# Smaller attention state, later weight loads, and the last stage's convolution split around the gate products

## What is computed

```python
# attention, b, h, block by block
out = (q @ k.T * Dmask) @ v + (q * lam_pow) @ kv_state
kv_state = lam ** block * kv_state + (k * rev_pow).T @ v
# experts: x is the attention output, e the token's expert
out[b, s] = p[e] * (np.maximum(x[b, s] @ w1[e], 0) @ w2[e])
# last layer
gate_pre = sum(conv_w[k] * xp[:, k:k + S, :] for k in range(5))
y = (sigmoid(gate_pre) * (x @ w_val)) @ w_out
```

## Time and profile before

| | |
|---|---|
| Time, median of 3 runs | 379.99 us (378.61 to 380.9) |
| The profiled execution | 382.69 us, span 380.9 us |
| PE busy | 358.0 us, 94% of the span |
| DVE, ACT, POOL busy | 236.8, 176.3, 70.7 us |
| Mean granted PE clock | 0.969 of full speed |

### The profile page before, as it was taken

How to read it: one execution, slowest core, us unless ns; L and a number is a source line. 1 busy time by engine, 2 the same in 40 slices (tenths; PEclk the granted TensorE clock), 3 DMA queues, 4 the chain that set the end, 5 groups by cost and what they waited for, 6 DMA issues and landing times.

```text
span 380.9 us, 6692 instructions
## 1 busy us (share of the span) xinstructions
PE 358.0 (94%) x2512; PEld 327.7 (86%) x2512; DVE 236.8 (62%) x511; ACT 176.3 (46%) x297; POOL 70.7 (19%) x66
## 2 busy tenths in 40 slices
PE   6997999979999999999999999999996993999997
PEld 5896999868998989899898998989995892998986
DVE  6776689986572672837647285571801889989420
ACT  1336256411263554636456274462620982955422
POOL 4426699872000000000000000000006600000000
PEclk9999699988999999999999999999999898799999
DMA  7999999336209476494755937464014600010113
GB/s 231 420 409 403 401 312 331 103 134 210 96 5 354 142 275 218 156 353 130 262 201 200 341 120 284 157 238 148 2 57 118 195 22 0 28 57 35 51 54 110
DMA packets 30761, 70.10 MB, mean 184 GB/s; under 512 B 2320, under 2 KB 2832, under 8 KB 30224
## 3 DMA queue, kind: packets, MB, share of 16 engines
q1 hardware_dynamic: 26192, 59.25, 43.9%
q0 software_dynamic: 1920, 6.29, 5.0%
q10 hardware_dynamic: 2624, 4.22, 3.0%
HBM read 55.08 MB, written 14.68 MB: 183 GB/s over the span
## 4 chain that ended last, share of the span: by engine, by line
PE 81%; DMA 8%; DVE 5%; ACT 3%; issue 2%; POOL 0%; SPq 0%; DVEq 0%; POOLq 0%
PE bank L1115 76%; DMA w_raw<-w 5%; DVE gate L1058 2%; PE bank L1268 2%; PE bank L1343 1%; PE bank L1168 1%; DMA y_slots<-y_out 1%; DMA x_all<-y_slots,gather_u 1%; DMA lam_all<-lam 1%; DVE decay L795 1%; PE bank L1185 1%; ACT gate L690 0%; ACT w_sp L676 0%; ACT w_raw L692 0%; ACT state_dec L565 0%
## 5 line engine op out<-in xcount | busy, mean ns | idle before, releaser
L1115 PE MATMUL bank<-w_sp,h_sp 128*128 128x512 f32 (+1 forms) x480 | 106.7, 380 | 0.0
L1115 PEld LDWEIGHTS bank<-w_sp,h_sp 128*128 128x128 f32 x480 | 86.3, 188 | 16.4
L1115 PEld LDWEIGHTS bank<-x_sp,w_sp 128*128 128x128 f32 x768 | 93.2, 192 | 0.9 <-issue 0.3
L1115 PE MATMUL bank<-x_sp,w_sp 128*128 128x256 f32 x768 | 93.8, 283 | 0.1
L898 DVE TENSOR_TENSOR w_sp<-w_raw,w_sp 128x1024 fp32r<-128x1024 f32 x60 | 70.8, 1222 | 12.3 <-ACT w_sp L556 12.1
L556 ACT ACTIVATE w_sp<-w_raw 128x1024 fp32r<-128x1024 f32 x68 | 68.6, 1057 | 16.8 <-PE bank L1115 13.6
L975 DVE SCALAR_TENSOR_TENSOR h_sp<-bank,h_sp 128x512 fp32r<-128x512 f32 x32 | 22.1, 690 | 63.6 <-ACT h_sp L596 62.6
L513 POOL DMA_INDIRECT x_all<-y_slots,gather_u x12 | 12.4, 1031 | 196.9 <-DMA y_slots<-y_out 193.6
L1115 PE MATMUL bank<-w_sp 128*128 128x384 f32 x192 | 37.9, 356 | 6.6 <-DVE prod L1073 6.6
L1115 PEld LDWEIGHTS bank<-w_sp 128*128 128x128 f32 x192 | 36.4, 204 | 7.9 <-DVE prod L1073 7.0
L596 ACT ACTIVATE h_sp<-bank 128x512 fp32r<-128x512 f32 x32 | 19.1, 597 | 48.1 <-PE bank L1115 48.1
(11 more groups left out here) (129 smaller groups left out, 402.6 us busy)
## 6 DMA issues: line engine op xcount, KB each, us to landing
w_raw<-w SPq DMA_DIRECT2D x32, 1024.0 KB, 5.8
qkv_sb<-qkv SPq DMA_DIRECT2D x22, 512.0 KB, 13.6
x_slots<-zeros SPq DMA_DIRECT2D x4, 1024.0 KB, 14.8
x_in<-x_slots SPq DMA_DIRECT2D x7, 512.0 KB, 6.7
y_slots<-y_out ACTq DMA_DIRECT2D x7, 512.0 KB, 5.3
out<-x_in SPq DMA_DIRECT2D x11, 256.0 KB, 2.0
w_raw<-w_val SPq DMA_DIRECT2D x1, 1024.0 KB
w_raw<-w_out SPq DMA_DIRECT2D x1, 1024.0 KB, 6.5
```

The lines of the kernel that those rows point to most:

```text
L1115: return nc.tensor.matmul(o, lhsT, rhs, start=start, stop=stop, skip_group_check=free)
```

## The change

**State.** The state of a pair is stored as 128 partitions by 64 columns, without the zeros: each head's block on its own 64 partitions. POOL's memset and the semaphore `state_zero` are gone, and DVE adds a whole tile's state in one instruction instead of two. In `between` and `keys_values` PE does one product per head instead of one per pair: 64 by 64 weights with 128 columns in the first, 128 by 64 weights with 64 columns in the second.

**Loads.** Expert 0's units are loaded with tiles 6 to 9 (UNITS_FROM = 6) and split from tile 5 on (SPLIT_FROM = 5). Expert 1's first three units are loaded after the loop over tiles. The last two halves are split by POOL at t = 12 and t = 13.

**Last layer.** `conv` can be called for some taps. For chunks 1 to 3 the taps of channel tiles 0 and 1 are done around `low_prod` of the chunk before, then two taps of tiles 2 and 3, then `gated` of tiles 0 and 1, then the other two taps. `project(k-1)` does two row tiles between the two halves of `values(k)` instead of one, except for the last chunk. ACT takes `high_yT(k+1)` and `scale_y(k+2)` first in its loop, and spreads `keep_yT(k+1)` and `keep_out`.

```diff
-SPLIT_FROM = 3
+SPLIT_FROM = 5
+UNITS_FROM = 6
...
-            state = sb_early("state", [P, B, PAIRS, P])
-            state_dec = sb_early("state_dec", [P, B, PAIRS, P])
+            state = sb_early("state", [P, B, PAIRS, D])
+            state_dec = sb_early("state_dec", [P, B, PAIRS, D])
...
-                if t - RING < RING:
-                    load_unit(0, t - RING)
-                if t >= TILES - 2:
-                    sp.wait_ge(lo_ok[t - TILES + 2], 2)
-                    load_unit(1, t - TILES + 2)
-            sp.wait_ge(lo_ok[2], 2)
-            load_unit(1, 2)
+                if 0 <= t - UNITS_FROM < RING:
+                    load_unit(0, t - UNITS_FROM)
+            for i in range(3):
+                sp.wait_ge(lo_ok[i], 2)
+                load_unit(1, i)
...
-            nc.gpsimd.memset(state[:, :, :, :], 0.0).then_inc(state_zero, 1)
...
+                half = t - SPLIT_FROM - 1
+                if t > TILES and half < 2 * RING:
+                    split_lo_half(half // 2, half % 2)
                 if t >= 3:
                     scatter(t - 3)
-                if SPLIT_FROM < t <= SPLIT_FROM + 2 * RING:
-                    split_lo_half((t - SPLIT_FROM - 1) // 2, (t - SPLIT_FROM - 1) % 2)
+                if 0 <= half and t <= TILES:
+                    split_lo_half(half // 2, half % 2)
...
             for k in range(1, CHUNKS):
-                for d in range(DT):
-                    sigmoid(k, d)
+                if k + 1 < CHUNKS:
+                    high_yT(k + 1)
+                if k + 2 < CHUNKS:
+                    scale_y(k + 2)
+                sigmoid(k, 0)
+                sigmoid(k, 1)
+                keep_out(k - 1, 0)
                 high_prod(k, 0)
                 high_prod(k, 1)
+                sigmoid(k, 2)
+                sigmoid(k, 3)
...
-                for s in range(2):
-                    r = slice(s * D, (s + 1) * D)
-                    if t >= B:
-                        last = nc.vector.tensor_tensor(state[r, b, :, r], kv[r, :, r], state_dec[r, b, :, r], ALU.add)
...
+                if t >= B:
+                    nc.vector.tensor_tensor(state[:, b], kv, state_dec[:, b], ALU.add).then_inc(state_ok, 1)
...
-            low_prod(0, (0, 1, 2, 3))
-            halo(1)
-            conv(1, (0, 1))
-            conv(1, (2, 3))
+            low_prod(0, (0, 1))
             for k in range(1, CHUNKS):
+                halo(k)
+                conv(k, (0, 1), (0, 1))
+                low_prod(k - 1, (2, 3))
+                conv(k, (0, 1), (2, 3))
+                conv(k, (2, 3), (0, 1))
                 gated(k, (0, 1))
+                conv(k, (2, 3), (2, 3))
                 low_prod(k, (0, 1))
...
-                    mm(ps_xT[:, a * P:(a + 1) * P], state[:, t % B, a, :], q_scaled[:, t % 2, a, :], a == 0, False, True)
+                    for s in range(2):
+                        r = slice(s * D, (s + 1) * D)
+                        mm(ps_xT[r, a * P:(a + 1) * P], state[r, t % B, a, :], q_scaled[r, t % 2, a, :],
+                           a == 0, False, True)
...
-                    last = mm(ps_kv[:, a * P:(a + 1) * P], k_scaled[:, t % 2, a, :], qkv_sb[:, t % RING, 3, a, :],
-                              True, True)
+                    for s in range(2):
+                        r = slice(s * D, (s + 1) * D)
+                        last = mm(ps_kv[r, a * D:(a + 1) * D], k_scaled[:, t % 2, a, r], qkv_sb[:, t % RING, 3, a, r],
+                                  True, True)
...
-                project(k - 1, (0,))
-                values(k, (2, 3))
-                project(k - 1, (1, 2))
+                if k + 1 < CHUNKS:
+                    project(k - 1, (0, 1))
+                    values(k, (2, 3))
+                    project(k - 1, (2,))
```

More of the change, by code:

```diff
@@ L1044, in halo, with conv @@
                 last.then_inc(halo_ok, 1)
-            def conv(k, tiles):
+            last_step = {}
+            def conv(k, tiles, taps=range(TAPS - 1)):
                 dve.wait_ge(halo_ok, k + 1)
                 src, dst = yT[k % 2], gate[k % 2]
-                last_step = {}
-                for n in range(TAPS - 1):
+                for n in taps:
                     for d in tiles:
@@ L1103, in _ @@
                     low_yT(k + 1)
-                    halo(k + 1)
-                    conv(k + 1, (0, 1))
                 gated(k, (2, 3))
-                low_prod(k, (2, 3))
-                if k + 1 < CHUNKS:
-                    conv(k + 1, (2, 3))
+            low_prod(CHUNKS - 1, (2, 3))
         @block.tensor
@@ L1389, in _ @@
                     transpose_y(k + 1)
[L1390 to L1392 removed]
+                if k + 1 < CHUNKS:
+                    project(k - 1, (0, 1))
+                    values(k, (2, 3))
+                    project(k - 1, (2,))
+                else:
+                    project(k - 1, (0,))
+                    values(k, (2, 3))
+                    project(k - 1, (1, 2))
             project(CHUNKS - 1, (0, 1, 2))
```

21 lines of the change are left out of this document (8 added, 13 removed).

## The result

The changed kernel takes 368.51 us (median of 4 runs, 366.58 to 369.39) beside 379.3 us of the kernel before (4 runs, 377.15 to 380.9): a ratio of 0.971, 95% interval 0.966 to 0.976. The forecast was 366.7 us with a range of 362.5 to 373.0. Every ratio in this text is to runs of the kernel before that were made beside it, and it leaves out runs more than 1.5% above the fastest of their kernel. The profiled execution takes 368.95 us (span 367.0 us) against 382.69 us (span 380.9 us).

What follows compares the result with a forecast made beforehand. PE's own work bounds a usual attention tile; waits and lost clock at tile 5 and in the last layer were recoverable. Terms -0.9 - 5.3 + 1.1 + 0.3 - 8.5 = -13.3 us gave 366.7 us (median), range 362.5 to 373.0.

Steps and rivals of the forecast that it cites:

- I take the same sum off both: Whole kernel: the forecast gain comes off both the profiled execution (382.69 us) and the median (379.99 us).
- Start, -0.9: Kernel start: without POOL's state memset, DVE's second copy and everything behind it start earlier; -0.9 us, range 0 to -0.94.
- Later weights, -5.3: Attention, tile 5 to 6: the wait for first weights and its clock loss go; -5.3 us, range -5.3 to -1.8.
- Rival (a): Attention, tiles 6 to 9: the loads bind again and give back 3.5 us, 370.2 us; chance 0.13.
- the prediction's own signs: Profile after: tiles at 6.0 to 6.1 us, clock 1.00 ahead of 75 us; wrong would be a tile above 6.4 us.
- State products, +1.1: Attention, `between` and `keys_values` done per head: +1.1 us over ten tiles, range -2.4 to +4.5.
- the loads alone fill the time, and the change loads the same weights: Attention, `keys_values`: weight loads rather than columns set its time, so +0.05 us per tile was taken.
- rival (d): Attention: columns set the time of `keys_values`, -2.4 us instead of +1.1, giving 363.2 us; chance 0.07.
- End of attention, +0.3: End of attention: DVE's split of the late tile may have to let POOL finish, up to 0.6 us; +0.3 taken.
- Last layer, -8.5: Last layer, chunk 1: PE's idle shrinks from 6.58 to 0.5 us and the clock stays; -8.5 us, range -9.0 to -5.5.
- Rival (b): Last layer: a longer wait keeps a cold stretch and the clock drops, 2.5 to 3 us back, 369.5 us; chance 0.10.
- Rival (e): State products: the two halves of a pair do not overlap, 21 us over ten tiles, 387 us, slower; chance 0.03.

Runs made afterwards that it cites:

- the kernel with the memset back: Changed kernel with a memset of the old size put back ahead of POOL's other start work, on an unused buffer: 370.66 us, ratio 0.981 to before.
- the zeros late: Changed kernel with the four 1 MB writes of zeros issued behind tiles 2, 3, 4 and 5: 366.66, 372.22, 374.00 and 374.74 us.
- the scatters behind them: Changed kernel with the writes of zeros late and POOL's first three scatters done together two tiles later: 365.91 us, ratio 0.965 to before.

## Why the prediction was right, and where its steps were not

*Total.* The forecast of the sum, -13.3 us, is near what the profiled executions show (-13.7 us), and part of that is luck. The four terms of the attention and its end were forecast at -0.9 - 5.3 + 1.1 + 0.3 = -4.8 us and came to -0.1 - 0.4 - 3.9 + 0.6 = -3.8 us, a new wait at tile 4 against cheaper products; and -1.6 us came from the fifth stretch, which the forecast did not have and which varies by more than that. The medians show -10.8 us, within the range. The step that failed for the median is the sentence "I take the same sum off both": the stall at tile 5 had taken the clock with it in the profiled execution of before (5.29 us), while the same stall cost 1.50 us in another execution of the same code, and its removal alone was worth 2.8 us. A term with clock in it may be taken whole off the execution that shows it, but not off the median. Whether this stall is also why that execution lay 2.7 us above the median is not shown: its mean clock, 0.969, is within what the other runs of before had.

*Start, -0.9.* Right at its place, PE's first `keys_values`: 10.07 - 9.23 = 0.84 us, with the mechanism it named. Little is left of it at tile 4, which starts 0.5 us earlier with the cheaper products counted in. What it is worth in the whole is open, see the kernel with the memset back. The prediction had tile 2's and 3's loads issued earlier "so the loads keep up"; they did not, since tile 4 was issued 1.44 us earlier and landed when it had before.

*Later weights, -5.3.* The mechanism was right: in the profile of the changed kernel ACT's first split has no wait for `w_raw`, and with this part alone tile 5 has no stall. The size was off for the median (2.8 us). Rival (a), a new wait for loads, came, but neither at tiles 6 to 9, where I had looked for it, nor between 30 and 60 us: it came at 28 us, at a tile whose load the change had not moved. I had not asked how near tile 4 was to its landing in the profile before. It was 0.5 us: its `scores` began at 28.63, its q and k were there at 28.1, and the change brings PE there 1.5 us sooner. In the profiled execution this cost 1.07 and 0.23 us of wait and some 1.5 us of clock. With it two of the prediction's own signs failed, a tile above 6.4 us (7.66) and a clock below 1.00 ahead of 75 us (0.66).

*State products, +1.1.* Wrong in sign. `between` came as said (1.02 us). `keys_values` took 0.62 us and not 0.94: this is the step that failed, "the loads alone fill the time, and the change loads the same weights". I let `logits`, with its 9 columns and 0.92 us, decide. But those loads are of 128 by 128 weights, and `keys_values` loads 16 times 64 columns, two halves side by side. The value was at the end of the range that I had worked out from columns (0.6), rival (d). With the tiled groups' cost to their neighbours the eight tiles that have both products are 0.10 us shorter each, and tiles 10 and 11, which have only `between`, 0.18 us longer each; so less than 1 us is won, where -2.4 us had been that rival's price. I had not counted the 0.05 to 0.07 us on each side of a tiled group. By the Trainium skill, TensorEngine Tiling (Array Packing), Key Properties, a change of tiling mode drains the engine. The rows agree in kind, but with three more changes per tile the tile grew by no more than 0.2 us besides `keys_values`, not by 0.6.

*End of attention, +0.3.* It was 0.46 us: DVE's split takes 1.15 us instead of 0.69, and PE's wait for it 0.89 us instead of 0.43. The trace had allowed 0 to 0.6 us; the Trainium skill, SBUF — State Buffer, Who interferes with whom, was right that it would be a full block: a VectorE instruction with both inputs in SBUF against a GpSimd instruction that reads SBUF. The runs show it twice, at `x_sp` and at `prob_e`.

*Last layer, -8.5.* Right in each number: idle 0.50 us (0.5 forecast), 24 products in 4.43 us (4.35), clock 1.00, no wait at `values(2)`. From `values(0)` to the end it is -8.5 us in the profiles, and about -7.6 us in the ratio of the kernel that has this part alone. Rival (b) did not come.

*Rival (e)*, that the halves do not overlap, is refuted by every tile.

What stays open: how often, and from what wait on, the clock falls. Waits of 1.07 (changed kernel) and 0.80 us (old order of PE) at tile 4 were followed by a clock of 0.66, waits of 0.92, 0.79, 0.75 and 0.62 us at the same place by 1.00. At tile 5 waits of 1.45 us (last layer alone) and 1.11 us (state alone) were followed by 1.00, and one of 1.11 us with the zeros late by 0.72 and 0.60.

## What to carry to other kernels

Before a gain is counted, look along the path for the next thing that it runs into: a transfer whose landing is fixed by the bytes ahead of it is one, and the slack in front of it (0.5 us here) is read from the trace before. A late transfer is cured by what stands ahead of it in the queue, and then whoever waits for what was moved has to move too: with the zeros moved alone three runs of four were some 4 to 6 us slower, with the scatters behind them the gain is 2.1 us. Price a stall with and without the clock that may go with it, and take only the part without it off a median.

## What the runs showed of the hardware

- Nearly the same wait may or may not be followed by the lower clock: at tile 4 1.07 us was followed by 0.66 and 0.92 us by 1.00, in two executions of the same kernel. The same attention code lost 5.29 us and 1.50 us at tile 5 in two executions, with clocks of 0.50 and 1.00 in the stretch behind the wait.
- Sixteen products of 64 columns, two side by side in the array, take 0.62 us where eight of 128 columns take 0.89 us; the full groups next to such a tiled group are 0.05 to 0.09 us longer.
- A memset by POOL holds a DVE copy of 64 by 4 elements until its end (1.5 us for two copies instead of 0.63), and a split by POOL holds DVE products with both inputs in SBUF until its end (0.69 to 1.15 us, 0.26 to 0.78 us).
